# A step of attention blocks woven into a gated MLP: another order on VectorE, and all value copies on ScalarE

## What is computed

```python
# 1: attention, 8 heads of 64; heads 0-3 see the last 32 positions, heads 4-7 every 32nd position
scores = scale * q @ k.T
scores = where(mask, scores, -1e9)
x = softmax(scores) @ v
# 2: gated MLP with a spatial mix
h = gelu_tanh(x @ w_in);  u, v = split(h)
v_n = layer_norm(v) * g_ln
v_s = w_sg @ v_n + b_sg
x = x + (u * v_s) @ w_out
# 3: feed-forward
out = x + relu(layer_norm(x) @ w_ch1) @ w_ch2
```

## Time and profile before

| | |
|---|---|
| time, median of 3 runs | 724.48 us (724.33 to 725.86) |
| the profiled execution | 724.19 us, span 722.4 us |
| TensorE busy | 97% of the span |
| VectorE, ScalarE, GpSimd busy | 46%, 34%, 27% |
| mean granted TensorE clock | 0.998 of full speed |

### The profile page before, as it was taken

The page is one execution under the profiler, slowest core; times in us unless marked ns, Lnnn a source line. Parts: engine busy times, 40 slices in busy tenths (PEclk is TensorE's granted clock), DMA queues, the critical chain, the costliest instruction groups (busy, mean ns, idle before and its releaser), DMA issues.

```text
span 722.4 us, 12879 instructions
## 1 busy us (share of the span) xinstructions
PE 703.0 (97%) x4766; PEld 668.5 (93%) x4768; DVE 329.7 (46%) x1032; ACT 248.3 (34%) x738; POOL 196.8 (27%) x194
## 2 busy tenths in 40 slices
PE   8899999998999899999999999999999999999998
PEld 4579888988898789999999999999999999999998
DVE  6877973598269835854532242214222222312112
ACT  6755762476146623524421211121122112111110
POOL 1377323322152247554250203022111302010000
PEclk9999999999999999999999999999999999999999
DMA  8560006000600010133401000000100010001001
GB/s 300 211 222 2 1 2 223 1 1 3 223 0 0 0 59 1 30 117 117 141 6 44 1 1 15 29 1 1 44 1 1 0 44 2 1 1 44 0 1 44
DMA packets 15992, 35.02 MB, mean 48 GB/s; under 512 B 1728, under 2 KB 5696, under 8 KB 15936
## 3 DMA queue, kind: packets, MB, share of 16 engines
q1 hardware_dynamic: 15936, 34.29, 13.6%
HBM read 29.56 MB, written 4.72 MB: 47 GB/s over the span
## 4 chain that ended last, share of the span: by engine, by line
PE 84%; DVE 7%; ACT 5%; issue 3%; DVEq 0%; ACTq 0%; POOL 0%; POOLq 0%
PE bank L950 26%; PE bank L952 26%; PE bank L951 26%; ACT probs L537 3%; DVE probs L747 3%; PE bank L1003 2%; DVE probs L734 1%; PE bank L974 1%; PE bank L987 1%; DVE gt L783 1%; DVE u_sb L787 1%; ACT probsT L547 1%; PE bank L958 1%; DVE stat L742 0%; ACT res L554 0%
## 5 line engine op out<-in xcount | busy, mean ns | idle before, releaser
L913 DVE SCALAR_TENSOR_TENSOR hid_lo<-bank,hid_hi 128x384 fp32r<-128x384 f32 x96 | 53.6, 558 | 280.6 <-ACT hid_hi L676 280.6
L676 ACT ACTIVATE hid_hi<-bank 128x384 fp32r<-128x384 f32 x96 | 47.1, 491 | 300.3 <-PE bank L952 300.3
L951 PE MATMUL bank<-xn_lo,w_hi 128*128 128x384 f32 x384 | 129.5, 337 | 0.0
L952 PE MATMUL bank<-hid_hi,w_lo 128*128 128x384 f32 x384 | 129.5, 337 | 0.0
L950 PE MATMUL bank<-hid_hi,w_hi 128*128 128x384 f32 x384 | 129.4, 337 | 0.0
L952 PE MATMUL bank<-xn_hi,w_lo 128*128 128x384 f32 x384 | 129.2, 336 | 0.0
L950 PE MATMUL bank<-xn_hi,w_hi 128*128 128x384 f32 x384 | 129.0, 336 | 0.0
L951 PE MATMUL bank<-hid_lo,w_hi 128*128 128x384 f32 x384 | 128.9, 336 | 0.0
L537 ACT ACTIVATE probs<-probs,stat 96x128 f32<-96x128 f32 (+2 forms) x192 | 71.9, 379 | 9.1 <-DVE stat L734 8.6
L950 PEld LDWEIGHTS bank<-hid_hi,w_hi 128*128 128x128 f32 x384 | 72.2, 188 | 0.0
L952 PEld LDWEIGHTS bank<-xn_hi,w_lo 128*128 128x128 f32 x384 | 72.1, 188 | 0.0
(11 more groups left out here) (97 smaller groups left out, 1304.7 us busy)
## 6 DMA issues: line engine op xcount, KB each, us to landing
w_raw<-w_ff_dram SPq DMA_DIRECT2D x16, 512.0 KB, 3.5
v_sb<-vW_dram SPq DMA_DIRECT2D x16, 384.0 KB, 7.1
k_sb<-kT_dram SPq DMA_DIRECT2D x15, 304.0 KB, 6.5
q_sb<-qT_dram SPq DMA_DIRECT2D x15, 288.0 KB, 6.2
out_dram<-res SPq DMA_DIRECT2D x5, 768.0 KB, 3.9
res<-w_sgT_dram SPq DMA_DIRECT2D x1, 1152.0 KB, 10.5
win_v_raw<-w_in_dram SPq DMA_DIRECT2D x4, 256.0 KB, 6.9
win_u_raw<-w_in_dram SPq DMA_DIRECT2D x4, 256.0 KB, 8.7
```

The source lines that it names most:

```text
L676: act.activation(hid_hi[:, f % 2, :], h_bank[f % 2][:, 0:TILE], ACT.Relu).then_inc(hh_ready, 1)
L913: dve.scalar_tensor_tensor(out=hid_lo[:, f % 2, :], in0=h_bank[f % 2][:, 0:TILE], scalar=0.0, in1=hid_hi[:, f % 2, :].bitcast(F32), op0=AL ...
L951: pe.matmul(dst, wh, xl, start=False, stop=False)
L952: last = pe.matmul(dst, wl, xh, start=False, stop=(stop and i == n - 1))
```

## The change

In a step, VectorE gates the second of the two MLP groups (2t) between the two normalisings and no longer behind both; `round_x` of head pairs 0 and 1 (steps 3 and 4) moves from before the normalisings to behind them; GpSimd does both `split_gated` of a step before `split_x`. All `copy_x` of the interleaved part are ScalarE's, so VectorE loses six copies in a pass (steps 3, 5, 7) and ScalarE gains them. Who waits for copies (`values`, `round_x`) waits for ScalarE's counter. The attention of sequence 0 keeps its alternation.

```diff
         def wait_copied(engine, b, s, quad=True):
 
-            by, n = (s // 2 % 2, s // 4 * 2 + s % 2) if quad else (s % 2, s // 2)
-            engine.wait_ge((x_act, x_dve)[by], b * (TWINS // 2) + (n + 1))
+            if quad:
+                engine.wait_ge(x_act, b * TWINS + (s + 1 - TWINS // 2))
+            else:
+                engine.wait_ge((x_act, x_dve)[s % 2], s // 2 + 1)
...
                     if 1 <= t <= NMIX // 2:
                         split_gated(b, 2 * t - 1)
+                    if t < NMIX // 2:
+                        split_gated(b, 2 * t)
                     if t in QUAD_X:
                         split_x(b + 1, QUAD_X[t])
-                    if t < NMIX // 2:
-                        split_gated(b, 2 * t)
...
                 for t in range(QUAD_STEPS):
-                    if t >= 2 and t % 2 == 0:
+                    if t >= 2:
                         copy_x(b + 1, 2 * t - 4)
                         copy_x(b + 1, 2 * t - 3)
...
                 for t in range(QUAD_STEPS):
-                    if t >= 2 and t % 2 == 1:
-                        copy_x(b + 1, 2 * t - 4)
-                        copy_x(b + 1, 2 * t - 3)
                     if t < QUADS:
                         maxima(b + 1, 2 * t)
                         maxima(b + 1, 2 * t + 1)
                     if t >= 1:
                         empty_group(b, 2 * t - 1)
-                    if t in QUAD_X:
+                    if t in QUAD_X and t >= QUADS:
                         round_x(b + 1, QUAD_X[t])
                     if t < QUADS:
                         normalise(b + 1, 2 * t)
+                    empty_group(b, 2 * t)
+                    if t < QUADS:
                         normalise(b + 1, 2 * t + 1)
-                    empty_group(b, 2 * t)
+                    if t in QUAD_X and t < QUADS:
+                        round_x(b + 1, QUAD_X[t])
                 empty_group(b, 2 * QUAD_STEPS - 1)
```

More of the change, by code:

```diff
@@ L748, in normalise, with copy_x @@
                 last.then_inc(probs_ready, 1)
[L750 to L753, removed]
+            def copy_x(s):
+                dst, src = heads_out(0, s)
+                dve.wait_ge(pv_ready, s + 1)
                 dve.tensor_copy(dst, src).then_inc(x_dve, 1)
@@ L759, in round_x @@
                 wait_copied(dve, b, last, quad)
-                wait_copied(dve, b, last - 1 - last % 2 if quad else last - 1, quad)
+                if not quad:
+                    wait_copied(dve, b, last - 1, quad)
                 settle(dve)
@@ L897, in _ @@
                 if s >= SOLO_LAG and s % 2 != SOLO_LAG % 2:
-                    copy_x(0, s - SOLO_LAG, quad=False)
+                    copy_x(s - SOLO_LAG)
                 if s % PER_PAIR == 0 and s >= 2 * PER_PAIR:
```

## The result

The changed kernel takes 714.3 us (median of 4 runs, 714.16 to 715.47); the kernel before, run beside it, takes 725.17 us (4 runs, 724.33 to 726.39). The ratio is 0.9852 with a 95% interval of 0.9832 to 0.9872, so 1.5% faster. The forecast was 715.0 us. The profiled execution took 714.38 us with a span of 712.6 us at a mean granted TensorE clock of 0.998, as before.

What follows compares the result with a forecast made beforehand. TensorE was taken as the bound, with 10.97 us of standstill to win. Passes gaining 3.37, 3.05 and 3.05 us sum to 9.5; 724.19 less that is 714.7, plus 0.3 for the median gives 715.0 us, range 713.2 to 718.8.

Steps and rivals of the forecast that it cites:

- The bound and the ceiling: TensorE, busy 97%, wins only from standstill in the steps: 3.87, 3.55 and 3.55 us a pass, 10.97 at most.
- (a): Second gate between normalisings: ScalarE loses its 2.06 us wait; GpSimd holds both normalisings, 1.54 us each instead of 1.00 free.
- the lead: VectorE's head start on TensorE in steps 1 to 5, second pass: 0.9, 0.5 and 0 to 0.1 us to spare.
- (b): VectorE's step sum: 6.60 us against TensorE's 6.45, no idle left, residual stall about 0.1 us.
- (c): GpSimd's split may catch a normalising's third multiply, 0.04 us ahead of it; 0.5 us a pass allowed, between 0.1 and 0.9.
- (d): ScalarE's added copies in steps 3, 5, 7 hide in freed waiting; uncovered, 0.42 to 0.7 us a step, 1.1 a pass.
- VectorE becomes the bound: Rival: held multiplies cost more than priced; 718 to 720 us. Chance 0.25 shared with ScalarE as the bound.
- (e): Late `round_x` and `split_x`: `split_x` falls under `maxima`, TensorE's 0.99 us wait in step 4 goes; zero cost.
- the step-4 mend: Rival: gate still late for ScalarE, only step 4's `split_x` mended; 1 of 3.55 us goes, 721 us; chance 0.04.
- Slower: Rival: longer GpSimd work holds both normalisings of each step, 2.75 us each; step 9.0 us, 740 us total; chance 0.03.
- unseen second hold: Condition for the slower rival: GpSimd work beyond one 0.8 us `split_gated` per normalising holding VectorE's multiplies.

Runs made afterwards that it cites:

- e5: Changed kernel with the second gate put back behind both normalisings; 723.09 us, 0.9972 of the kernel before.
- e11: Kernel before with the gate moved, and GpSimd's even splits and `split_x` waiting until the second normalising is done; 715.18 us, 0.9848 of before.
- e12: The changed kernel run once more, unaltered, beside the late-split version on one chip; 714.46 us, 0.9839 of the kernel before.
- e2: Kernel before with only the copies of `values` in the steps all moved to ScalarE; 722.12 us, 0.9952 of before.
- e4: Changed kernel with the copies of `values` shared between ScalarE and VectorE as before; 718.57 us, 0.9913 of the kernel before.
- e3: Kernel before with only `round_x` moved behind the normalisings and `split_x` behind both splits; 724.32 us, 0.9981 of before.
- e1: Kernel before with only the second gate of each step moved between the two normalisings; 729.39 us, 1.0061 of before.
- e10: Changed kernel with `round_x` and `split_x` back in their old places; 726.35 us, 1.0008 of the kernel before.
- e9: Changed kernel with a useless second GpSimd subtraction ahead of each `split_gated` of the steps; 716.62 us, 0.9868 of the kernel before.

## Why the prediction came out right

*The bound and the ceiling.* The measure (standstill between equal pieces, 10.97 us) held: 9.70 us of it were won, and the rest lies in the first pass. The unstalled 30.67 of a pass came out to the hundredth, by luck: I had 6.45 for each of steps 1 to 3 and 5.66 for steps 4 and 5, and the steps took 6.45, 6.47, 6.29, 5.77 and 5.69. So step 3 hid 0.16 us more standstill than I read from it, and steps 4 and 5 had 0.14 less.

*(a) The gate between the normalisings.* Right in its mechanism, and e5 and e11 show it from both sides: without it 2.5 us of a pass stay, with it and a quiet GpSimd next to none. ScalarE's rounding waits 0.48 us in step 2. The price of a held normalising, 1.54, measured 1.55 (reciprocal at 144.03, gate behind the multiplies at 145.58). I had noted that the new place puts GpSimd under both normalisings of each step. In steps 1 and 2 it does, and this was harmless only by the lead. In steps 3 and 4 it doesn't: the second normalisings run free (multiplies 0.79 at 159.64 and 0.84 at 165.37), where I had put a held one.

*(b) VectorE's step.* 6.60 predicted, 6.61 and 6.62 measured for steps 1 and 2, against TensorE's 6.45. Step 3 takes 6.06 (154.66 to 160.72) and not the 6.62 of my working, for the reason just given, so the lead had more in hand than I counted. The lead lasts in the second and third passes (standstill 0, predicted 0.1). In the first it doesn't. I worked the lead out for the second pass and gave the first the same, with 0.5 us of standstill where 1.27 and 1.67 (e12) were measured: that step failed. GpSimd's weight splits hold the first normalising there, and VectorE starts without a lead. The rival "VectorE becomes the bound" is true in that one pass, where TensorE's steps are 6.55 to 6.61.

*(c) The edge of the third multiply.* The mis-sized term. I allowed 0.5 us a pass, 1.5 in all, mostly for a split that would catch the third multiply. It never did in the steps that I read: the multiply kept a lead of 0.03 us, where I had worked out 0.04. Measured: 0 in two passes. That the sum was nearly right (9.5 against 9.70) is partly luck, since the 1.27 us that the first pass lost, for another reason, took the place of 1.5. Some luck is in the time too: the medians fell by 10.9 us, and the 715.0 was met to 0.7 because the kernel before, which I had at 724.48, was measured at 725.17 this time.

*(d) The copies.* Hidden, as predicted; they cost 0.44 us in e2, where they have no cover (0.42 predicted for that). What I hadn't seen is that VectorE, rid of them, also moves against GpSimd (e2), and that 0.8 us of the later passes hang on the time that they free (e4).

*(e) `round_x` and `split_x`.* TensorE's wait of 0.99 us is gone. But I put its value at 1 us by itself and called it the step-4 mend; e3 gives 0.6 us in the second and third passes, and e1 and e10 show what it is for: with the gate moved and these two in their old places, `split_x` meets the normalisings of steps 3 and 4, and these passes stand still for 2.8 to 5.0 us in place of 0 to 0.8.

*The rivals.* "Slower" was priced on two normalisings of 2.75 us a step. e1_gate has just such normalisings, from 161.66 to 164.41, one each in steps 3 and 4, and it is slower than before. I had called that an unseen second hold; it was in plain sight as `split_x`, and the one thing that keeps the change from it is (e). What the prediction had no term for is the clock: in e1 and e10 a stall of 1.6 us could cost another 1.54.

The edits don't add up. Standstill in the second pass: before 3.55; gate 5.00; copies 2.56; `round_x` 2.93; the last two 2.57; gate and copies 4.36; gate and `round_x` 0.80; all three 0. Added singly (+1.45, -0.99, -0.62) they would leave 3.39.

## What to carry to other kernels

Where an engine waits for a result that itself waits for that engine's earlier work, the order inside the step can be worth more than any single duration; but move it only with a list of what GpSimd will then run under which VectorE instruction, since here each GpSimd instruction that began while multiplies were still to come cost one held multiply, but for the near ties below. Judge the parts of such a change together, since one alone may lose what the whole wins, and say for each pass what lead the late engine starts with.

## What the runs showed of the hardware

- *The hold is per instruction.* A VectorE multiply that waits under a GpSimd instruction ran when that one ended, even if another GpSimd instruction stands right behind (0.85 us in e9 with 1.6 us of GpSimd). In before and e1 two in a row held two multiplies, 2.6 us for four.
- *GpSimd waits too, and who gets through in a near tie isn't settled.* In step 3 of the changed kernel a multiply begins at 160.18, 0.10 behind GpSimd's subtraction, and runs in its free 0.26, as does the cast behind it; here GpSimd waits, and its 0.8 us become 1.39. The multiply of 144.64 began 0.03 us ahead of GpSimd and ran free, but the first multiply of 161.35 before the change, also 0.03 ahead (161.38), took 0.90. Single instructions of DVE and POOL, changed kernel, step 3:

```profile
160.18 0.26 DVE L749 TENSOR_SCALAR probs<-probs,stat 90x90 f32<-90x90 f32 x1
160.35 0.45 DVE L764 CAST xop_hi<-res 128x576 fp32r x1
...
160.08 1.39 POOL L418 TENSOR_TENSOR gated_lo<-u_sb,gated_hi 128x288 fp32r<-128x288 f32 x1 [1.55 <-ACT gated_hi L585]
```

- *The granted clock fell in the middle of a pass*, to 0.50 of 2.4 GHz, in e1 behind a stretch in which TensorE was busy for 0.87 of 2.48 us. One fall cost 1.54 us in e10, where the same program had it in two passes and not in the third.
- *The start scatters, and mostly with the clock.* The first scores of the steps came between 62.68 and 65.39 us in 14 profiles, although no edit changes the work ahead of them. The windows of PE in that part (as above; first the changed kernel, then e3) show falls of the granted clock in different places:

```profile
24.00:28.00 4.00, 3.35 (x31) 1.00 1.03 366
40.00:44.00 4.00, 4.00 (x11) 0.57 0.70 219
...
24.00:28.00 4.00, 2.99 (x10) 0.53 1.02 361
28.00:32.00 4.00, 4.00 (x27) 0.61 0.06 20
```

The six profiles with one fall, between 36 and 44 us, have 62.68 to 63.02. The seven with a longer fall at 24 to 32 us, or with two, at 24 to 32 and at 40 to 48, have 63.84 to 65.39. e12 has no fall there and still 63.38, so something else moves the start too, and that stays open. Spans that differ by 2 us say nothing here without the distance between two points inside the program.
